# Attention's rows ahead of its keys, the zeroth feature in four runs, a normalisation on ScalarE and two mirrored sums on GpSimd, in a fused attention and two-MLP kernel

## The chip, the cores and the metric

One NeuronCore of a Trainium2 chip runs the kernel. The metric is device microseconds of one execution, median over runs. An engine is named as in the profile: PE is TensorE, PEld its weight loads, DVE is VectorE, ACT is ScalarE, POOL is GpSimd, SP is SyncE, which here only issues transfers.

## The reference, cut to what matters

```python
# attention with decay, B=2, H=8, S=768, D=64, blocks of 64 positions
for b in range(nb):
    intra = einsum(einsum(qb, kb) * Dmask, vb)
    inter = einsum(qb * lam_pow, kv_state)
    out[:, :, sl] = intra + inter
    kv_state = lam_block * kv_state + einsum(kb * rev_pow, vb)
x = out as (B, S, 512)
u = x + real(fft(fft(x, axis=1), axis=2))
x = u + relu(norm(u) @ w_ch1) @ w_ch2            # 512 -> 2048 -> 512
out = x + relu(norm(x) * g_ln @ w_ch1') @ w_ch2'
```

All is float32 from outside. `norm` subtracts the mean of a row and divides by its deviation.

## The kernel before

The program is written out by hand: each engine has one list of instructions in a fixed order, and semaphores join them. An engine that waits holds everything behind it in its list.

**Attention.** Six blocks `c` of 128 tokens, two batches `b`, so 12 units `u = 2c + b`. For a unit PE computes the scores (`scores_of`), DVE multiplies them by the decay mask (`masks`), PE makes the rows (`rows`: the state's part and the masked scores times values; it needs the values, the queries that POOL has multiplied by powers, and the masks), and PE makes keys times values for the state (`keys_values`; it needs POOL's decayed keys `kd`). DVE adds these to the state (`grow_state`), ACT spreads the state (`expand`) and copies the rows out (`x_rows`). In the order before, `keys_values` stands ahead of `rows` in each unit of the loop. SP loads block `c` in two parts, queries and keys (`load_qk`, L301) and keys and values by token (`load_kv`, L304), each 1 MB, and behind each part 512 KB of the first MLP's weights, then the Fourier constants `C1` (L341). PE also runs 11 + 24 matmuls on zeros at the start (L486, L491).

**Fourier stage.** `along(f, c)` (L527) is the transform along the tokens, 16 features of three matmuls each; ACT copies each out (`y_columns`, L848). The column of feature zero is computed apart by small matmuls in `zeroth_feature` (L548), one after each of the 15 `along` of f = 3 to 7, with outputs of 128, 64 or 1 partitions and two columns. `features` (L591) is the transform along the features. DVE forms sums and differences (`differences`) and adds half of them to U (`add_mirrored`, L1202), POOL the other half (`add_rows`, L1581).

**MLPs.** 48 pairs `n`, eight to a stage `s`, six stages: three groups of 512 tokens for each MLP. A pair is seven products of 256 columns (L647), six matmuls each, and 24 matmuls of 512 columns of the second layer (L667) for the pair before it, `down(n - 1, half, t)`. `down(n - 1, 1, 0)` comes right behind the third product of pair n. It waits for the low halves of the second weights of chunk n - 1 (`down_lo`, L1158, on DVE in stage 0) and of the hidden values (`hidden_lo`, L1306). ACT copies the first, seventh and sixth product out (L927, L932, L944), splits weights (`up_hi` L818 and L820, `down_hi` L839) and the next stage's input (`x_hi`, L899), and makes `hidden_hi` (L915). During stage s the input of stage s + 1 is prepared: `statistics`, `deviation` (L864, on ACT), `row_scale`, `normalise` (L1271), in the second MLP also a product with `g_ln` on POOL (`scale_rows`, L1537), then sums (`x_sum`) and the split.

What the program prints for the functions that the diff touches:

## Time and profile before

| | |
|---|---|
| median of 3 runs | 584.7 us (583.88 to 584.91) |
| profiled execution, its own time | 584.5 us |
| its span, first to last instruction | 582.5 us |
| PE busy | 568.9 us, 98% |
| DVE, ACT, POOL busy | 353.3, 242.7, 162.7 us |

The span leaves 2.0 us of the execution outside it. PE is busy for all but 13.6 us of the span. A busy time says that an engine executes, not how much of the array its matmuls use: the small matmuls of the zeroth feature count as the large ones do.

### The profile page before, as it was taken

What the parts mean: (1) busy time and instruction counts of PE and PEld (TensorE: products, weight loads), DVE (VectorE), ACT (ScalarE), POOL (GpSimd) and SP (SyncE); (2) the same over time, 40 slices, a digit from 0 to 9 for tenths busy, and PEclk for the clock granted to TensorE, in tenths of its full rate; (3) what the DMA queues carried; (4) which work ended last, traced back from release to release, by engine and by line L of the source; (5) the groups of instructions that cost most, each with busy time, mean ns of one, the idle gap of its engine ahead of it and who ended that gap; (6) DMA issues with size and microseconds to landing.
All of it is one profiled execution on the core that took longest, in us unless ns stands there. A gap on an engine that the chain in (4) does not pass through costs nothing.

```text
span 582.5 us, 10727 instructions
## 1 busy us (share of the span) xinstructions
PE 568.9 (98%) x4037; PEld 390.6 (67%) x4037; DVE 353.3 (61%) x627; ACT 242.7 (42%) x475; POOL 162.7 (28%) x143
## 2 busy tenths in 40 slices
PE   8999999999899999999999999899999999999997
PEld 4889978666566666666666666566666666666663
DVE  3437788998875775646878676674265433422223
ACT  1255567546663234323546554363222342323231
POOL 1568931763710011003286312620003400000000
PEclk9999999999999999999999999999999999999999
DMA  7999981000137436531235522132000123100001
GB/s 239 393 378 377 351 264 55 2 20 0 37 56 193 132 111 154 136 91 38 74 90 113 141 74 73 36 55 55 19 2 2 37 55 109 73 2 1 0 1 72
DMA packets 78515, 59.85 MB, mean 103 GB/s; under 512 B 39418, under 2 KB 65666, under 8 KB 77060
## 3 DMA queue, kind: packets, MB, share of 16 engines
q1 hardware_dynamic: 76260, 54.49, 32.3%
q10 hardware_dynamic: 1728, 3.15, 1.4%
q0 software_dynamic: 480, 1.57, 0.9%
q8 instruction: 31, 0.51, 0.4%
q14 instruction: 16, 0.13, 0.1%
HBM read 43.73 MB, written 6.30 MB: 86 GB/s over the span
## 4 chain that ended last, share of the span: by engine, by line
PE 77%; DVE 9%; DMA 5%; issue 5%; POOL 3%; ACT 1%; DVEq 0%; SPq 0%; ACTq 0%; POOLq 0%
PE bank L667 36%; PE bank L647 32%; DMA arena<-attn 4%; PE bank L527 2%; PE bank L478 2%; DVE arena L1306 1%; DVE arena L1151 1%; PE bank L473 1%; DVE arena L1149 1%; POOL arena L1479 1%; DVE arena L1158 1%; PE bank L443 1%; PE bank L456 1%; PE bank L591 1%; DVE arena L1271 1%
## 5 line engine op out<-in xcount | busy, mean ns | idle before, releaser
L667 PE MATMUL bank<-arena 128*128 128x512 f16 x1152 | 287.2, 379 | 3.2 <-DVE arena L1158 3.1
L647 PE MATMUL bank<-arena 128*128 128x256 f16 x2016 | 259.3, 273 | 2.7 <-issue 1.9
L647 PEld LDWEIGHTS bank<-arena 128*128 128x128 f16 x2016 | 196.4, 98 | 78.0 <-issue 3.8
L667 PEld LDWEIGHTS bank<-arena 128*128 128x128 f16 x1152 | 112.2, 98 | 90.4 <-DVE arena L1158 3.9
L1306 DVE SCALAR_TENSOR_TENSOR arena<-arena 128x512 f16<-128x512 f32 x96 | 74.2, 773 | 62.4 <-ACT arena L915 62.2
L915 ACT ACTIVATE arena<-arena 128x512 f16<-128x512 f32 x96 | 60.4, 629 | 98.3 <-DVE arena L1353 92.9
L1347 DVE SCALAR_TENSOR_TENSOR arena<-bank,arena 128x256 f32<-128x256 f32 x48 | 20.3, 422 | 65.1 <-PE bank L647 64.7
L1537 POOL TENSOR_TENSOR arena<-arena 128x512 f32<-128x512 f32 x12 | 18.6, 1570 | 90.0 <-DVE arena L1271 90.0
L960 ACT ACTIVATE arena<-bank 128x256 f32<-128x256 f32 x48 | 18.3, 381 | 52.8 <-PE bank L647 52.7
L1283 DVE TENSOR_TENSOR arena<-arena 128x512 f16<-128x512 f32 x42 | 33.0, 796 | 10.1 <-ACT arena L899 10.1
L1353 DVE SCALAR_TENSOR_TENSOR arena<-bank,arena 128x256 f32<-128x256 f32 x48 | 20.2, 421 | 27.4 <-PE bank L647 27.4
L1517 POOL TENSOR_TENSOR arena<-arena 128x256 f32<-128x256 f32 x16 | 14.1, 883 | 80.8 <-DMA arena<-w 64.0
L932 ACT ACTIVATE arena<-bank 128x256 f32<-128x256 f32 x48 | 18.4, 383 | 41.7 <-PE bank L647 41.7
L944 ACT ACTIVATE arena<-bank 128x256 f32<-128x256 f32 x48 | 18.4, 383 | 38.7 <-PE bank L647 38.6
L927 ACT ACTIVATE arena<-bank 128x256 f32<-128x256 f32 x48 | 18.2, 379 | 30.5 <-PE bank L647 30.5
L899 ACT ACTIVATE arena<-arena 128x512 f16<-128x512 f32 x42 | 25.6, 624 | 12.3 <-POOL arena L1537 12.1
L1329 DVE SCALAR_TENSOR_TENSOR arena<-bank,arena 128x256 f32<-128x256 f32 x48 | 20.1, 419 | 17.2 <-PE bank L647 16.8
L478 PE MATMUL bank<-arena 128*128 128x64 f32 x192 | 26.2, 264 | 0.7 <-DVE arena L1034 0.7
L1149 DVE SCALAR_TENSOR_TENSOR arena<-arena 128x1024 f16<-128x1024 f32 x16 | 24.5, 1534 | 2.3 <-ACT arena L818 2.3
L478 PEld LDWEIGHTS bank<-arena 128*128 128x128 f32 x192 | 24.8, 192 | 1.2 <-issue 1.1
L1034 DVE TENSOR_TENSOR arena<-bank,arena 128x512 f32<-128x512 f32 x24 | 15.3, 682 | 13.5 <-PE bank L443 13.5
L1158 DVE SCALAR_TENSOR_TENSOR arena<-arena 128x1024 f16<-128x1024 f32 x16 | 23.2, 1451 | 0.0
(108 smaller groups left out, 527.1 us busy)
## 6 DMA issues: line engine op xcount, KB each, us to landing
arena<-w SPq DMA_DIRECT2D x48, 256.0 KB, 4.3
arena<-w SPq DMA_DIRECT2D x24, 512.0 KB, 4.5
arena<-attn SPq DMA_DIRECT2D x10, 1024.0 KB, 8.9
out<-arena SPq DMA_DIRECT2D x12, 256.0 KB, 2.3
arena<-attn SPq DMA_DIRECT2D x4, 512.0 KB, 4.2
x_near<-arena ACTq DMA_DIRECT2D x6, 256.0 KB, 7.5
x_far<-arena ACTq DMA_DIRECT2D x6, 256.0 KB, 6.2
arena<-c SPq DMA_DIRECT2D x1, 1153.5 KB, 12.1
```

Of the source, the lines that this page charges most:

```text
L478: last = nc.tensor.matmul(xps[b][:, h * D:(h + 1) * D], PT[b][:, par, pair, :], v, start=first, stop=True, skip_group_check=not first)
L647: last = nc.tensor.matmul(bank_, wst[:, i, wx, w, kt, :], xs[s % 2][:, x, ux, :, kt, :], start=not started and k == 0, stop=k == 5, skip_g ...
L667: last = nc.tensor.matmul(ops[t][:], hT[n % 2][:, half, hx, t * P:(t + 1) * P], wdn[:, i, wx, half * DM:(half + 1) * DM], start=first and ...
L899: nc.scalar.activation(hi, block_, ACT.Copy).then_inc(xh_done, 1)
L915: nc.scalar.activation(hT[n % 2][:, half, 0, :], z[n % 2][:, half, :], ACT.Relu).then_inc(hh_done, 1)
L1149: nc.vector.scalar_tensor_tensor(lo[:, 0:1024], sums, scale, hi[:, 0:1024], ALU.mult, ALU.subtract)
L1158: nc.vector.scalar_tensor_tensor(wdn[:, c, 1, :], raw, wscale[:, 2 * m + 1:2 * m + 2], wdn[:, c, 0, :], ALU.mult, ALU.subtract).then_inc(w ...
L1283: nc.vector.tensor_tensor(lo, block_, hi, ALU.subtract).then_inc(xl_done, 1)
L1306: nc.vector.scalar_tensor_tensor(hT[n % 2][:, half, 1, :], z[n % 2][:, half, :], 0.0, hT[n % 2][:, half, 0, :], ALU.max, ALU.subtract).the ...
L1329: nc.vector.scalar_tensor_tensor(z[n % 2][:, 0, 0:HT], chain[1 - n % 2], H_SCALE, p1, ALU.mult, ALU.add).then_inc(z11_out, 1)
L1347: nc.vector.scalar_tensor_tensor(z[n % 2][:, 1, 0:HT], seventh[:, 0:HT], H_SCALE, u2, ALU.mult, ALU.add).then_inc(z21_out, 1)
L1353: nc.vector.scalar_tensor_tensor(z[n % 2][:, 1, HT:TOK], a, H_SCALE, p7, ALU.mult, ALU.add).then_inc(z22_out, 1)
```

## The change

What it does, in the order of the program: the zero matmuls between the first scores and the rows are 21 in place of 24. The mask's two halves arrive on semaphores of their own, the first rows use the first half as soon as it is multiplied, and ACT in place of DVE copies the mask's column `kcol`. In each unit `rows` stands ahead of `keys_values`. The zeroth feature is four runs of three matmuls with four columns each (both batches and both parities at once), behind the `along` of f = 3, 4, 5 and 7, of 128, 128, 128 and 1 output partitions. The columns of `C1` are reordered for it. ACT splits the first half of chunk 1 ahead of `y_columns(5)`, with a wait for `x_out[0]` alone. In stage 0 the two last mirrored sums (j = 4, 5) are on POOL, `down_lo(0, i)` stands directly behind `hidden_lo(n, 1)`, and the input of stage 1 is normalised by ACT in pair 4 (`normal`), as scale times value plus `shift`, a new DVE instruction in `row_scale`. In the stage s = 3 `x_hi` of `X_SECOND` stands behind `hidden_hi(n, 1)` on ACT.

```diff
-WARM_BEFORE, WARM_BETWEEN = 11, 24
+WARM_BEFORE, WARM_BETWEEN = 11, 21
-ZEROTH = ((0, 1, 129, 0, 128, 0), (1, 64, 192, 0, 128, 2), (0, 129, 193, 0, 64, 4), (1, 0, 64, 64, 128, 4),
-          (0, 0, 1, 0, 1, 6))
+ZEROTH = {3: (1, 129, 0), 4: (257, 385, 4), 5: (129, 257, 8), 7: (0, 1, 12)}
...
@@ sync @@
-                             ).then_inc(mask_in, 16)
+                             ).then_inc(mask_in[par], 16)
@@ tensor: rows @@
-                pe.wait_ge(mask_done, 2 * u + 2)
...
+                if first:
+                    for par in range(2):
+                        pe.wait_ge(mask_done, 2 * u + 1 + par)
+                        for pair in range(PAIRS):
+                            last = values(pair, par)
+                else:
+                    pe.wait_ge(mask_done, 2 * u + 2)
...
@@ tensor: the units @@
             rows(0, 0, 0, True)
+            rows(0, 1, 0, True)
             keys_values(0, 0, 0, True)
-            rows(0, 1, 0, True)
...
                     pe.wait_ge(kv_in[slot], 16 * i + 16)
+                    rows(c, 0, slot, False)
                     keys_values(c, 0, slot, False)
-                    rows(c, 0, slot, False)
 
                     scores_of(0, 1 - slot, next_arrived, 4 * c + 2)
+                    rows(c, 1, slot, False)
                     keys_values(c, 1, slot, False)
-                    rows(c, 1, slot, False)
...
@@ tensor: the zeroth feature @@
-            def zeroth_feature(k, c):
-
-                par, lo, hi, first, end, at = ZEROTH[k]
-                return nc.tensor.matmul(bank[7][first:end, at:2 + at], C1[:, c, par * NE + lo:par * NE + hi],
-                                        zeroth_rows[:, par, :] if c == 0 else sfold[(HALF + c) % 2][:, :, par, 0],
-                                        start=c == 0, stop=c == HALF - 1)
+            def zeroth_feature(f):
+
+                lo, hi, at = ZEROTH[f]
+                for c in range(HALF):
+                    if f == 3 and c == HALF - 1:
+                        pe.wait_ge(sf_done, B * HALF)
+                    column = zeroth_rows if c == 0 else sfold[(HALF + c) % 2][:, :, :, 0].rearrange("p b q -> p q b")
+                    last = nc.tensor.matmul(bank[7][0:hi - lo, at:4 + at], C1[:, c, lo:hi], column,
+                                            start=c == 0, stop=c == HALF - 1)
+                if f == 7:
+                    last.then_inc(zeroth_done, 1)
...
                     for c in range(HALF):
                         last = along(f, c)
-                        if f == 3 and c == HALF - 1:
-                            pe.wait_ge(sf_done, B * HALF)
-                        if f < 8:
-                            zeroth = zeroth_feature(f - 3, c)
                     last.then_inc(f1_done, 1)
-                    if f == 7:
-                        zeroth.then_inc(zeroth_done, 1)
+                    if f in ZEROTH:
+                        zeroth_feature(f)
...
@@ scalar @@
+            for par in range(2):
+                act.wait_ge(mask_in[par], 16)
+                last = nc.scalar.activation(kcol.rearrange("p (a r) -> p a r", r=2)[:, :, par], DT[:, par, :, 0], ACT.Copy)
+            last.then_inc(kcol_done, 1)
...
+            def normal(tiles):
+
+                act.wait_ge(shift_done, 1)
+                for t in tiles:
+                    nc.scalar.activation(un[:, t, :], U[:, NT + t, :], ACT.Identity, bias=shift[:, t:t + 1],
+                                         scale=rs[:, t:t + 1]).then_inc(un_done, 1)
...
                 nc.scalar.activation(p1, a, ACT.Copy, scale=H_SCALE).then_inc(p1_out, 1)
...
+                if n == 4:
+                    normal((0, 1))
                 act.wait_ge(p7_done, n + 1)
                 act.wait_ge(z22_out, n)
                 nc.scalar.activation(p7, seventh[:, 0:HT], ACT.Copy, scale=H_SCALE).then_inc(p7_out, 1)
...
+                if n == 4:
+                    normal((2, 3))
                 if prep is not None:
-                    if i == late + 2:
+                    if i == late + 2 and s > 0:
                         deviation(prep)
...
                 nc.scalar.activation(u2, a, ACT.Copy, scale=H_SCALE).then_inc(u2_out, 1)
-                if prep is not None:
+                if n == 3:
+                    deviation(1)
+                if prep is not None and s != GROUPS:
                     for k in X_SECOND[late].get(i, ()):
                         x_hi(prep, k)
...
                 hidden_hi(n, 1)
+                if s == GROUPS:
+                    for k in X_SECOND[late].get(i, ()):
+                        x_hi(prep, k)
...
             y_columns(4)
+            act.wait_ge(x_out[0], 16)
+            up_hi(0, 1, (0,))
             y_columns(5)
             y_columns(6)
-            for b in range(B):
-                act.wait_ge(x_out[b], 16)
-            up_hi(0, 1, (0,))
             y_columns(7)
...
@@ vector @@
-            dve.wait_ge(mask_in, 32)
-            for par in range(2):
-                last = nc.vector.tensor_copy(kcol.rearrange("p (a r) -> p a r", r=2)[:, :, par], DT[:, par, :, 0])
-            last.then_inc(kcol_done, 1)
...
+                    if u == 0:
+                        dve.wait_ge(mask_in[par], 16)
...
+                if s == 1:
+                    dve.wait_ge(ln_step, step + 7)
+                    nc.vector.scalar_tensor_tensor(shift, mv[:, :, 0], -1.0, rs, ALU.mult, ALU.mult).then_inc(shift_done, 1)
...
-                if n == 4:
-                    add_mirrored(5)
...
+                if s == 0:
+                    down_lo(0, i)
                 if prep is not None:
...
                     if i == late + 2:
                         row_scale(prep)
-                        normalise(prep, (0, 1))
+                        if s > 0:
+                            normalise(prep, (0, 1))
                     for k in X_SECOND[late].get(i, ()):
                         x_lo(prep, k)
-                if s == 0:
-                    down_lo(0, i)
...
-                if n == 3:
-                    add_mirrored(4)
...
-                    if i == late + 2:
+                    if i == late + 2 and s > 0:
                         normalise(prep, (2, 3))
...
@@ gpsimd @@
+            def add_mirrored(j):
+
+                pool.wait_ge(ub_in[1], 16 * 6)
+                for half in range(2):
+                    u = U[:, 2 * j + 1, 256 * half:256 * half + 256].rearrange("p (m e) -> p e m", e=2)
+                    last = nc.gpsimd.tensor_tensor(u, u, mirror(DE[DE_SLOT[j]][:, 1 - half, :], half), ALU.add)
+                last.then_inc(addC, 1)
...
             add_rows(4)
+            add_mirrored(4)
             up_sums(0, 5)
             add_rows(5)
+            add_mirrored(5)
             up_sums(0, 6)
```

DVE in pair 3, before, from `hidden_lo(3, 1)` (L1306) on; L1255 to L1264 are `row_scale`, L1271 is `normalise`, L1158 `down_lo`, L1202 `add_mirrored`:

```order
L1306 SCALAR_TENSOR_TENSOR arena<-arena 128x512
L1255 RECIPROCAL arena<-arena 128x4
L1257 TENSOR_TENSOR arena<-arena 128x4
L1259 TENSOR_TENSOR arena<-arena 128x4
L1261 TENSOR_SCALAR arena<-arena 128x4
L1264 TENSOR_TENSOR arena<-arena 128x4
L1271 TENSOR_SCALAR arena<-arena 128x512 x2
L1158 SCALAR_TENSOR_TENSOR arena<-arena 128x1024
L1306 SCALAR_TENSOR_TENSOR arena<-arena 128x512
L1202 TENSOR_TENSOR arena<-arena 128x2x128 x2
L1271 TENSOR_SCALAR arena<-arena 128x512 x2
```

and in the changed kernel, from the same instruction (L1344; L1191 is `down_lo`, L1302 the new `shift`, L1367 the first eviction of pair 4):

```order
L1344 SCALAR_TENSOR_TENSOR arena<-arena 128x512
L1191 SCALAR_TENSOR_TENSOR arena<-arena 128x1024
L1290 RECIPROCAL arena<-arena 128x4
L1292 TENSOR_TENSOR arena<-arena 128x4
L1294 TENSOR_TENSOR arena<-arena 128x4
L1296 TENSOR_SCALAR arena<-arena 128x4
L1299 TENSOR_TENSOR arena<-arena 128x4
L1302 SCALAR_TENSOR_TENSOR arena<-arena 128x4
L1344 SCALAR_TENSOR_TENSOR arena<-arena 128x512
L1367 SCALAR_TENSOR_TENSOR arena<-bank,arena 128x256
```

`down_lo` has moved ahead of `row_scale`; four `normalise` and two halves of a mirrored sum are gone, one small instruction is new.

ACT in pair 4 before, from the copy of the first product (L927); L899 is `x_hi`, L818 and L820 `up_hi`:

```order
L927 ACTIVATE arena<-bank 128x256
L932 ACTIVATE arena<-bank 128x256
L944 ACTIVATE arena<-bank 128x256
L899 ACTIVATE arena<-arena 128x512
L818 ACTIVATE arena<-arena 128x1024
L820 ACTIVATE arena<-arena 128x768
L915 ACTIVATE arena<-arena 128x512
```

and in the changed kernel (L954, L961 and L975 are the copies of the first, seventh and sixth product, L925 is `normal`, L919 `x_hi`):

```order
L954 ACTIVATE arena<-bank 128x256
L925 ACTIVATE arena<-arena 128x512 x2
L961 ACTIVATE arena<-bank 128x256
L925 ACTIVATE arena<-arena 128x512 x2
L975 ACTIVATE arena<-bank 128x256
L919 ACTIVATE arena<-arena 128x512
L834 ACTIVATE arena<-arena 128x1024
L836 ACTIVATE arena<-arena 128x768
```

Two normalisations stand ahead of the copy of the seventh product and two ahead of that of the sixth.

ACT in pair 27 (the fourth pair of stage 3) before, from the copy of the sixth product:

```order
L944 ACTIVATE arena<-bank 128x256
L899 ACTIVATE arena<-arena 128x512
L818 ACTIVATE arena<-arena 128x1024
L820 ACTIVATE arena<-arena 128x768
L915 ACTIVATE arena<-arena 128x512
L960 ACTIVATE arena<-bank 128x256
L915 ACTIVATE arena<-arena 128x512
```

and in the changed kernel:

```order
L975 ACTIVATE arena<-bank 128x256
L834 ACTIVATE arena<-arena 128x1024
L836 ACTIVATE arena<-arena 128x768
L942 ACTIVATE arena<-arena 128x512
L919 ACTIVATE arena<-arena 128x512
L996 ACTIVATE arena<-bank 128x256
L942 ACTIVATE arena<-arena 128x512
```

`x_hi` (L899 before, L919 now) stood ahead of `up_hi` and `hidden_hi` and now stands behind both.

## Rows read from the trace of the kernel before

**Rows 1.** The view of the cores: span and mean granted TensorE clock.

```profile
core 0: 582.5 us, clock 0.999
```

**Rows 2.** Page, part 1: busy us, share and instructions of each engine.

```profile
PE 568.9 (98%) x4037; PEld 390.6 (67%) x4037; DVE 353.3 (61%) x627; ACT 242.7 (42%) x475; POOL 162.7 (28%) x143
```

**Rows 3.** Waits of PE: us in total, times, longest us.

```profile
PE bank L667 <- DVE arena L1158: 3.1, 3, 1.8
PE bank L456 <- POOL arena L1479: 2.0, 5, 0.5
```

**Rows 4.** Timeline of PE, attention: start us, us, what, [idle before].

```profile
1.32 4.21 PE L486 MATMUL bank<-arena 128*128 128x512 f16 x11 [1.32 <-POOL arena L1454]
...
7.45 5.35 PE L491 MATMUL bank<-arena 128*128 128x512 f16 x24
...
15.90 0.69 PE L456 MATMUL bank<-arena 128*64 128x64 f32 x16 [0.48 <-POOL arena L1479]
...
34.77 1.16 PE L443 MATMUL bank<-arena 64*128 64x128 f32 x16
...
53.62 1.16 PE L443 MATMUL bank<-arena 64*128 64x128 f32 x16
...
65.06 3.20 PE L527 MATMUL bank<-arena 128*128 128x193 f32 x18
```

**Rows 5.** Timeline of SP's queue: start us, us of issuing, what.

```profile
22.49 2.38 SPq L301 DMA_DIRECT2D arena<-attn  x1
...
45.48 0.38 SPq L301 DMA_DIRECT2D arena<-attn  x1
...
50.88 2.34 SPq L341 DMA_DIRECT2D arena<-c  x1
```

**Rows 6.** Transfers issued in 22 to 23 us: KB, median us to landing.

```profile
arena<-attn SPq DMA_DIRECT2D x1, 1024.0 KB, 11.4
```

**Rows 7.** The same for 45.2 to 45.6 us.

```profile
arena<-attn SPq DMA_DIRECT2D x1, 1024.0 KB, 7.3
```

**Rows 8.** Page, part 6, the same for the whole span.

```profile
arena<-c SPq DMA_DIRECT2D x1, 1153.5 KB, 12.1
```

**Rows 9.** A window: us, busy PE, PEld, DVE, ACT, POOL; PEclk; DMA share; GB/s.

```profile
30.00:50.00 20.00, 19.17 (x240) 17.82 (x238) 10.04 (x19) 10.99 (x22) 12.46 (x9) 1.00 1.07 373
```

**Rows 10.** Timeline of PE, zeroth feature and after.

```profile
68.50 0.59 PE L527 MATMUL bank<-arena 128*128 128x192 f32 x2
...
71.81 0.57 PE L527 MATMUL bank<-arena 128*128 128x192 f32 x2
...
76.17 0.59 PE L527 MATMUL bank<-arena 128*128 128x192 f32 x2
...
78.56 3.71 PE L591 MATMUL bank<-arena 128*128 128x257 f32 x16 [0.39 <-ACT arena L848]
...
83.15 8.08 PE L527 MATMUL bank<-arena 128*128 128x193 f32 x48
```

**Rows 11.** Timeline of DVE, pairs 2 to 4.

```profile
127.43 1.27 DVE L1240 BATCH_NORM_STATS2 arena<-arena 128x6 f32<-128x512 f32 x2
...
136.52 0.69 DVE L1306 SCALAR_TENSOR_TENSOR arena<-arena 128x512 f16<-128x512 f32 x1
...
138.13 1.00 DVE L1271 TENSOR_SCALAR arena<-arena 128x512 f32<-128x512 f32 x2
139.04 1.28 DVE L1158 SCALAR_TENSOR_TENSOR arena<-arena 128x1024 f16<-128x1024 f32 x1
...
150.31 1.74 DVE L1158 SCALAR_TENSOR_TENSOR arena<-arena 128x1024 f16<-128x1024 f32 x1
```

**Rows 12.** Timeline of PE, the down matmuls of pair 4.

```profile
140.38 0.82 PE L667 MATMUL bank<-arena 128*128 128x512 f16 x3 [0.50 <-DVE arena L1158]
```

**Rows 13.** Timeline of ACT, pair 27.

```profile
375.70 0.63 ACT L899 ACTIVATE arena<-arena 128x512 f16<-128x512 f32 x1 [5.53 <-POOL arena L1537]
```

**Rows 14.** Timeline of PE, pair 28.

```profile
379.08 1.47 PE L647 MATMUL bank<-arena 128*128 128x256 f16 x12 [1.94 <-issue]
```

51 lines of the change are left out of this document (31 added, 20 removed).

## The prediction

> **What bounds the kernel now.** First the view of the cores: the span is 582.5 us at a mean granted clock of 0.999, so TensorE runs at the upper of its two levels, 2.4 GHz [rows 1]. Then the page's first part: PE is busy for 568.9 us of it, 98%, and no other engine for more than 61% [rows 2]. So only two things can shorten the kernel: fewer or cheaper matmuls, or some of the 13.6 us in which PE is idle. The waits of PE name the largest idle pieces: 3.1 us in three waits of the down matmuls for `down_lo`, and 2.0 us in five waits of `keys_values` for POOL's decayed keys [rows 3]. The timelines add three: 1.94 us in pair 28 [rows 14], 0.39 us ahead of `features` [rows 10], 1.32 us at the start [rows 4]; most of the rest lies behind the last matmul, which the change does not touch. The reader should then ask of each piece not who releases it, but what is late next when that releaser is no longer waited for.
>
> **Attention: rows ahead of keys.** The sum of what could go is the 2.0 us of [rows 3], that is 0.48 us in the first unit [rows 4] and about 0.4 in each of four blocks. The wait is for kd, a POOL product of the block's keys, made after the keys land. With `rows` first PE needs only the landing, and POOL works under `rows`. But this stage has a second limit close behind. In 30 to 50 us the DMA engines show a busy share of 1.07 at 373 GB/s [rows 9], and the queue holds a backlog: a queries and keys part issued at 22.49 us [rows 5] lands after 11.4 us [rows 6], at 33.9; PE first uses it at 34.77 [rows 4], 0.9 us later. For the last block it is 45.48 [rows 5] and 7.3 us [rows 7], so 52.8, used at 53.62 [rows 4]: 0.8 us. I take a backlog as the sign that a landing depends on the bytes ahead of it and not on when it is issued; then these landings stay where they are while PE moves up, and the next `scores_of` waits for them. So the gain of the whole stage is capped by that slack, **0.8 us**. The start gains nothing beside it: the split mask and three fewer zero matmuls (24 take 5.35 us [rows 4], 0.22 each, so 0.7) only bring PE earlier to the keys that are at 15.90 now, and these wait for a landing and POOL, which do not move. `C1` lands at 50.88 + 12.1 = 63.0 us [rows 5, 8]; PE would want it at 65.06 - 0.8 = 64.3 [rows 4], so it is not late. Bounds: 0 if PE keeps the transfers' pace with its slack unspent, 2.6 (the 2.0 and 0.6 of the start) if the landings follow PE.
>
> Keys that come behind rows make the state later by the 0.6 to 0.7 us of `keys_values` [rows 4] plus a DVE sum and ACT's copy, but it is used two units later, which is about 9 us (34.77 to 53.62 are four units, 4.7 each [rows 4]). I cost it at nothing. `kcol` on ACT is hidden by the same late keys.
>
> **The zeroth feature.** In [rows 10] the six steps of f = 3 and 4 take 71.81 - 68.50 = 3.31 us, 0.552 each; the next six 76.17 - 71.81 = 4.36, 0.727 each; the last three up to 78.56 - 0.39 = 78.17 take 2.00, 0.667 each. An `along` by itself costs 8.08 / 24 = 0.337 [rows 10]. So a small matmul costs 0.215 with a full output, 0.39 with 64 partitions and 0.33 with one: 1.29 + 2.34 + 0.99 = 4.6 us. Afterwards nine have a full output, 9 x 0.215 = 1.94. Four columns in place of two should cost nothing, since two cost 0.215 and 192 only 0.337. The three with one partition stand at the end and run while PE would wait 0.39 us for ACT anyway; I take 0.5 for the larger of both. So 68.50 to 78.56, 10.06 us, becomes 15 x 0.337 + 1.94 + 0.5 = 7.5: **gain 2.6 us**, 2.0 if the last three cost their 0.33 each and the full ones stop hiding anything, 2.7 at best. ACT's fourth small copy and the earlier half of chunk 1 lie beside this. Everything behind, DVE's chain from `differences(0)` to the first normalisation too, starts from `features` and moves with it.
>
> **Stage 0.** The three waits are 3.1 us: 0.8, 0.50 [rows 12] and 1.8 [rows 3]. In each `down_lo` came last. Now it goes ahead of two statistics (1.27 us [rows 11]) in pair 2. In pair 3 `hidden_lo` is through at 137.1 and `down_lo` began at 139.04 [rows 11]: it can move up by 1.9 us, the wait was 0.50. In pair 4 it ran behind an `x_lo` and, beside POOL, took 1.74 us in place of 1.28 [rows 11]; the DVE work ahead of it is lighter by four normalisations (0.5 each) and two mirrored sums. So most of the three go. What is late next: POOL now has 3 us more of work in pairs 2 and 3, and ACT has four normalisations at the price of an `x_hi`, 0.63 [rows 13] and about 0.55 when they follow each other. They can start only when `shift` is there: 137.1 + 1.2 for `down_lo` + 1.0 for `row_scale` + 0.2 = 139.5. Two take until 140.6, the copy of the seventh product until 141.0. PE would be at the first down matmul at 140.38 - 0.50 - 0.8 = 139.1, and needs that copy three groups of matmuls later, each 3 x 0.22 = 0.66: at 141.0. That is no slack at all, and the second two normalisations before the sixth product's copy are as tight. I put 0.4 us there, 0.4 for what POOL's neighbourhood leaves of the three waits: **gain 2.3 us**, from 3.1 down to 1.3.
>
> At this place a row and a rule meet. The same `down_lo` took 1.28 and 1.74 us [rows 11], the longer one beside POOL. The Trainium skill, "GPSIMD Engine Reference", Specifications, says why: GpSimd shares its SBUF interface with VectorE, and DVE instructions with two SBUF inputs contend. The trace agrees in 0.46 us. By that rule moving two sums to POOL does not free all the DVE time it seems to: it is the third rival.
>
> **Stage 3.** ACT's `x_hi` for the next stage waited 5.53 us for POOL's product with `g_ln`, until 375.70 [rows 13], and held `hidden_hi(27, 1)` and the last copy of pair 27 behind it; PE stood for 1.94 us at the second product of pair 28 [rows 14]. Now `hidden_hi` is ahead. The copy is still behind `x_hi`: it can start at 375.70 + 0.55 = 376.3 and be through at 376.7, and PE needs it where its wait begins, 379.08 - 1.94 = 377.1. **Gain 1.9 us**; bounds 0.5, if something else holds the copy, and 1.94.
>
> **Sum.** 0.8 + 2.6 + 2.3 + 1.9 = 7.6 us. Against the profiled execution's 584.5 that is 576.9; its time is 0.2 us under the median of 584.7, so the forecast is **577.1 us**, by itself within 576.1 to 578.3.
>
> **Rivals.**
> The transfers follow PE (14%): if a landing is a fixed time behind its issue, the 2.6 us are all gained. The two landings that I use took 11.4 and 7.3 us [rows 6, 7], which speaks against a fixed time, as does the busy share of 1.07. 575.3 us.
> Attention gains nothing (12%): the small transfers to DRAM from ACT come earlier and push the loads back by the slack. 577.9.
> Stage 0 gives back (16%): POOL beside DVE delays `down_lo`, `row_scale` and so the normalisations on ACT by 1 us, and PE waits that much at the fourth product of pair 4, and for `down_lo` as before in part. 3.1 shrinks to a gain of 0.9: 578.5.
> The clock falls (6%): in the changed order both units' rows of block 0 are through about 1.5 us before the keys at 15.90, so PE idles there longer than the 0.48 us now [rows 4]. At the start eleven matmuls took 4.21 us, 0.38 each, against 0.22 later [rows 4], so the lower level is near half the pace. If that phase came back for as long, 4.2 us of time would do 2.1 us of work: 577.1 + 2.1 = 579.2. The Trainium skill, "TensorE: Matmul & The Clock Gate", Part 1, warns of exactly this, that an idle PE goes back to half its clock; no row here has an idle piece of that length within the work, so the trace neither agrees nor disagrees.
> The zeroth runs are not cheap (4%): in a run each matmul must load its weights with nothing beside it. If each of twelve costs 0.35, the 2.6 shrinks to 1.0: 578.7.
> The other side (3%): the state is late. If `keys_values` behind `rows` made `grow_state`, `expand` and the next rows of the same batch a chain, every one of the 8 units in blocks 2 to 5 would wait; from 7.6 / 8 = 0.95 us each it eats the whole gain, and at 1.2 us the time is 586.7. The two units between speak against it.
> The forecast has 45%.
>
> **Range and chances.** 574.9 to 580.0 takes in the transfers that follow, stage 0 at its worst and the clock; some 15% stay outside. A measurement of this kernel tells about 0.2% (1.2 us) from no change. Faster by more than that 95%, within it 2%, slower 3%.
>
> **What would show it.** In the trace of the changed kernel: POOL no longer named for `keys_values`, and in its place waits of about 0.4 us of `scores_of` for the transfer of queries and keys in each block; the first `along` at 64.3 us (62.5 if the transfers follow); `features` at 75.1 to 75.3 us; in pair 4 a PE wait under 0.5 us on ACT's normalisations; no wait in pair 28; all other pairs as long as before. A first `along` later than 65.1, a granted clock under 0.99 before 30 us, or a wait over 1 us in pairs 2 to 5 would make it wrong.

## The result, and the profile after

The changed kernel takes **581.54 us** (median of 20 runs, 579.83 to 585.2) against 584.56 us of the kernel before (20 runs beside it); the ratio is 0.9954, with a 95% interval of 0.9943 to 0.9966. That is 2.7 us faster by the ratio, where 7.6 us had been forecast. The profiled execution took 582.56 us, with a span of 580.8 us at a mean granted clock of 0.995, against 582.5 us at 0.999 before [rows 1].

First the page of the changed kernel: the span, the busy times, the granted clock over 40 slices, and one row of the DMA queues.

```profile
span 580.8 us, 10716 instructions
...
PE 567.3 (98%) x4028; PEld 390.7 (67%) x4028; DVE 360.9 (62%) x618; ACT 246.2 (42%) x483; POOL 167.2 (29%) x147
...
PEclk9999999998999999999999999999999999999999
...
q8 instruction: 32, 0.52, 0.4%
```

PE is busy for 1.6 us less than before [rows 2] and idle for 13.5 us, nearly as long as before: waits went, and others came. The tenth digit of PEclk is an 8, where the clock was lower for a time. The mean of 0.995 holds a second such time: from 578.4 us to the end of the span the granted clock is 0.5 as well, but PE's last matmul has ended by then and nothing is slowed. In the kernel before that time is 0.9 us long, here 2.4, since the last output lands later (below).

Now PE's timeline in the places of which the prediction speaks: attention, the zeroth feature and what is behind it, and pairs 3 to 5.

```profile
17.04 1.16 PE L445 MATMUL bank<-arena 64*128 64x128 f32 x16 [0.64 <-DMA arena<-attn]
...
20.83 0.48 PE L486 MATMUL bank<-arena 128*128 128x128 f32 x2 [0.92 <-ACT arena L793]
...
75.40 3.71 PE L602 MATMUL bank<-arena 128*128 128x257 f32 x16 [0.29 <-ACT arena L864]
...
90.11 1.06 PE L643 MATMUL bank<-arena 128*128 128x128 f32 x8 [0.30 <-DVE arena L1309]
...
94.67 0.81 PE L658 MATMUL bank<-arena 128*128 128x256 f16 x6 [0.42 <-DVE arena L1321]
...
134.55 2.14 PE L658 MATMUL bank<-arena 128*128 128x256 f16 x18 [0.28 <-DVE arena L1184]
...
140.94 0.96 PE L658 MATMUL bank<-arena 128*128 128x256 f16 x6 [1.99 <-ACT arena L961]
...
148.47 2.13 PE L658 MATMUL bank<-arena 128*128 128x256 f16 x18
```

`features` starts at 75.40, 3.16 us earlier than at 78.56 [rows 10], and pair 0 at 94.67, 2.66 us earlier than at 97.33. Up to here it is nearly as forecast. But pair 4 then takes 148.47 - 134.55 = 13.92 us, and before it took 10.44 (137.75 to 148.19). In it stands a wait of 1.99 us for ScalarE's copy of the seventh product (L961).

ScalarE and VectorE in pairs 3 and 4 say what the copy stood behind. L925 is `normal`, L1182 and L1184 are `up_lo`, L1191 is `down_lo`, L1290 to L1302 are `row_scale` with `shift` at its end.

```profile
139.09 1.52 ACT L925 ACTIVATE arena<-arena 128x512 f32<-128x512 f32 x2 [3.29 <-DVE arena L1302]
140.52 0.36 ACT L961 ACTIVATE arena<-bank 128x256 f32<-128x256 f32 x1
...
131.24 1.84 DVE L1182 SCALAR_TENSOR_TENSOR arena<-arena 128x1024 f16<-128x1024 f32 x1 [0.33 <-ACT arena L834]
133.01 1.49 DVE L1184 SCALAR_TENSOR_TENSOR arena<-arena 128x768 f16<-128x768 f32 x1
134.42 0.68 DVE L1344 SCALAR_TENSOR_TENSOR arena<-arena 128x512 f16<-128x512 f32 x1
135.02 1.75 DVE L1191 SCALAR_TENSOR_TENSOR arena<-arena 128x1024 f16<-128x1024 f32 x1
136.69 0.17 DVE L1290 RECIPROCAL arena<-arena 128x4 f32<-128x4 f32 x1
136.89 0.48 DVE L1292 TENSOR_TENSOR arena<-arena 128x4 f32<-128x4 f32 x1
137.41 0.65 DVE L1294 TENSOR_TENSOR arena<-arena 128x4 f32<-128x4 f32 x1
138.09 0.17 DVE L1296 TENSOR_SCALAR arena<-arena 128x4 f32<-128x4 f32 x1
138.29 0.57 DVE L1299 TENSOR_TENSOR arena<-arena 128x4 f32<-128x4 f32 x1
138.89 0.17 DVE L1302 SCALAR_TENSOR_TENSOR arena<-arena 128x4 f32<-128x4 f32 x1
```

ScalarE is idle for 3.29 us until `shift` is there at 139.06, then normalises two tiles, and only then copies. GpSimd works beside all of this: its mirrored sums (L1625), and from 134.63 to 138.85 us the four sums of the next chunk of weights, chunk 6 (L1553 to L1558):

```profile
131.26 2.42 POOL L1625 TENSOR_TENSOR arena<-arena 128x256 f32<-128x256 f32 x2
134.63 1.05 POOL L1553 TENSOR_TENSOR arena<-arena 128x256 f32<-128x256 f32 x1 [0.95 <-DVE arena L1184]
135.65 1.71 POOL L1554 TENSOR_TENSOR arena<-arena 128x256 f32<-128x256 f32 x1
137.31 0.72 POOL L1556 TENSOR_TENSOR arena<-arena 128x256 f32<-128x256 f32 x1
138.12 0.73 POOL L1558 TENSOR_TENSOR arena<-arena 128x256 f32<-128x256 f32 x1
```

The three VectorE operations of 0.48, 0.65 and 0.57 us end at 137.37, 138.06 and 138.86, each within 0.03 us of the end of one of these sums (137.36, 138.03, 138.85).

In the kernel before that first sum (L1517) came much later, held by VectorE's mirrored sum of pair 4 (L1202):

```profile
143.68 0.72 POOL L1517 TENSOR_TENSOR arena<-arena 128x256 f32<-128x256 f32 x1 [9.73 <-DVE arena L1202]
```

The busy times by windows show what came behind the wait (behind the window and its length stand PE, PEld, DVE, ACT and POOL, then the granted clock, the DMA share and GB/s).

```profile
138.00:141.50 3.50, 1.51 (x12) 0.82 (x11) 1.89 (x6) 2.41 (x5) 0.77 (x2) 1.00 0.00 0
141.50:144.90 3.40, 3.40 (x14) 1.70 (x12) 0.83 (x3) 3.40 (x6) 1.27 (x1) 0.50 0.00 0
144.90:148.00 3.10, 3.10 (x18) 1.67 (x17) 3.10 (x5) 2.22 (x5) 0.82 (x1) 1.00 0.00 0
```

From 141.49 to 144.91 us the granted clock is 0.5, that is 1.2 GHz: 3.4 us of time for 1.7 us of work.

The last loss is behind the work. PE's last matmul was 3.85 us earlier than before, the end of the span only 1.74 us. These are two rows of the DMA view of the changed kernel around its last output transfer: the queue of instructions with its packets, MB and share, and one transfer's median time from issue to landing.

```profile
q8 instruction: 1, 0.02, 2.1%
...
out<-arena SPq DMA_DIRECT2D x1, 256.0 KB, 4.2
```

And the same view of the kernel before, around its last transfer, where no row of a queue of instructions stands:

```profile
out<-arena SPq DMA_DIRECT2D x1, 256.0 KB, 2.1
```

In the changed kernel a read of 16 KB in the queue of instructions starts at 576.57 us, 0.44 us behind the issue of the last transfer, and takes 1.66 us. The last of the transfer's sixteen parts lands at 580.34, the fifteen others from 578.03 to 578.21. Before, the sixteen landed within 0.18 us.

The profiled execution as a sum (each row but the last is a difference of PE's starts in the two traces):

| part | forecast | measured |
|---|---|---|
| attention, first `along` 65.06 to 64.29 | 0.8 | 0.77 |
| zeroth feature, up to `features` | 2.6 | 2.39 |
| `features` to pair 0 | 0 | -0.50 |
| stage 0, pairs 0 to 5: 62.59 to 63.57 us | 2.3 | -0.98 |
| stage 3, pair 28: 11.92 to 9.76 us | 1.9 | 2.16 |
| behind the last matmul | 0 | -2.10 |
| sum | 7.6 | 1.7 |

### The profile page after: what moved, and what is told of

Read it like the earlier page. It is cut to its first block, busy times and chain, and to the rows that moved or that the text cites. A ratio compares the mean times of both kernels' runs of the same rounds, so it can differ in the third digit from the quotient of the medians.

```text
span 580.8 us, 10716 instructions
## 1 busy us (share of the span) xinstructions
PE 567.3 (98%) x4028; PEld 390.7 (67%) x4028; DVE 360.9 (62%) x618; ACT 246.2 (42%) x483; POOL 167.2 (29%) x147
## 4 chain that ended last, share of the span: by engine, by line
PE 74%; DVE 10%; DMA 5%; issue 4%; POOL 2%; SPq 2%; ACT 1%; DVEq 0%; ACTq 0%; POOLq 0%
PE bank L678 36%; PE bank L658 32%; DMA arena<-attn 5%; PE bank L537 1%; DVE arena L1182 1%; DVE arena L1344 1%; DVE arena L1184 1%; PE bank L475 1%; PE bank L486 1%; PE bank L445 1%; DVE arena L1191 1%; DVE arena L1235 1%; DVE arena L1309 1%; SPq L271 1%; DVE arena L1275 1%
## 5 line engine op out<-in xcount | busy, mean ns | idle before, releaser
L1344 DVE SCALAR_TENSOR_TENSOR arena<-arena 128x512 f16<-128x512 f32 x96 | 73.6, 767 | 59.0 <-ACT arena L942 58.9
L1321 DVE TENSOR_TENSOR arena<-arena 128x512 f16<-128x512 f32 x42 | 33.9, 817 | 10.7 <-ACT arena L919 10.6
L1553 POOL TENSOR_TENSOR arena<-arena 128x256 f32<-128x256 f32 x16 | 15.5, 971 | 74.6 <-DMA arena<-w 64.7
L961 ACT ACTIVATE arena<-bank 128x256 f32<-128x256 f32 x48 | 18.4, 383 | 40.7 <-PE bank L658 40.7
L975 ACT ACTIVATE arena<-bank 128x256 f32<-128x256 f32 x48 | 18.4, 384 | 36.2 <-PE bank L658 36.2
L954 ACT ACTIVATE arena<-bank 128x256 f32<-128x256 f32 x48 | 18.3, 380 | 30.4 <-PE bank L658 30.4
L1367 DVE SCALAR_TENSOR_TENSOR arena<-bank,arena 128x256 f32<-128x256 f32 x48 | 20.1, 419 | 16.5 <-PE bank L658 16.5
L919 ACT ACTIVATE arena<-arena 128x512 f16<-128x512 f32 x42 | 25.6, 622 | 7.2 <-POOL arena L1573 7.2
L1182 DVE SCALAR_TENSOR_TENSOR arena<-arena 128x1024 f16<-128x1024 f32 x16 | 26.9, 1682 | 0.6 <-ACT arena L834 0.6
L1191 DVE SCALAR_TENSOR_TENSOR arena<-arena 128x1024 f16<-128x1024 f32 x16 | 23.7, 1482 | 0.3 <-ACT arena L855 0.3
L1111 DVE TENSOR_REDUCE arena<-arena 128x1 f32<-128x1024 f32 x18 | 21.8, 1211 | 0.7 <-DMA arena<-w 0.7
```

Source lines behind the costliest of these rows:

```text
L919: nc.scalar.activation(hi, block_, ACT.Copy).then_inc(xh_done, 1)
L1111: nc.vector.tensor_reduce(wmax_chunks[:, m, c:c + 1], raw, AX.X, ALU.max, apply_absolute_value=True).then_inc(wred[m], 1)
L1182: nc.vector.scalar_tensor_tensor(lo[:, 0:1024], sums, scale, hi[:, 0:1024], ALU.mult, ALU.subtract)
L1191: nc.vector.scalar_tensor_tensor(wdn[:, c, 1, :], raw, wscale[:, 2 * m + 1:2 * m + 2], wdn[:, c, 0, :], ALU.mult, ALU.subtract).then_inc(w ...
L1321: nc.vector.tensor_tensor(lo, block_, hi, ALU.subtract).then_inc(xl_done, 1)
L1344: nc.vector.scalar_tensor_tensor(hT[n % 2][:, half, 1, :], z[n % 2][:, half, :], 0.0, hT[n % 2][:, half, 0, :], ALU.max, ALU.subtract).the ...
```

## The experiments

All ratios are to the kernel before, run beside each kernel. "Pairs 3, 4, 5" are their lengths in the profiled execution: 10.75, 10.44 and 11.73 us in the kernel before, 10.21, 13.92 and 9.76 in the changed one.

### Four kernels from the changed one

**Normalisations one place later.**

```diff
-                if n == 4:
-                    normal((0, 1))
                 act.wait_ge(p7_done, n + 1)
...
                 if n == 4:
-                    normal((2, 3))
+                    normal((0, 1))
...
                 if n == 3:
                     deviation(1)
+                if n == 4:
+                    normal((2, 3))
```

> The changed kernel with ScalarE's four normalisations of the second stage one place later in pair 4: tiles 0 and 1 behind the copy of the seventh product instead of ahead of it, tiles 2 and 3 behind the copy of the sixth. Theory (W): what the changed kernel loses in pair 4 (13.92 us long against 10.44) is TensorE's wait of 1.99 us for the seventh copy, queued behind normalisations that wait for shift until 139.06, and the granted clock of 0.5 that follows this idle time for 3.41 us and costs about 1.7 us. Then here no wait over 0.7 us stands in pair 4, the clock stays at 1.00 past 141 us, pair 4 takes 10.0 to 10.7 us, and the median is 2.5 to 3.7 us under the changed kernel's, 577.9 to 579.0. Rival (P): GpSimd's work beside VectorE holds up pair 4 whoever normalises; then pair 4 stays over 12 us, and the time within 1 us of the changed kernel's. Rival (C): the clock falls in this stage whatever TensorE waits; then only the 1.99 us come back and a stretch at 0.5 stands somewhere between 125 and 160 us.

Ratio 0.9935 (0.9921 to 0.9950), 580.93 us. Pairs 3, 4, 5: 10.21, 11.74, 10.08. The wait of 1.99 us is gone, the longest in pair 4 is 0.68 us, and the clock is 1.00 in all the work. Of the 3.5 us lost in pair 4, 2.2 came back, and 0.3 were lost again in pair 5. Theory W holds for the wait of 1.99 us, but pair 4 was to be 10.7 at most and the median 579.0 at most: `shift` is as late as in the changed kernel (139.24), and the place on ScalarE does not decide that.

**Stage 0's edits undone, the sums left on GpSimd.** The square root (`deviation`) goes back to its place too.

```diff
-                if n == 4:
-                    normal((0, 1))       # scalar, and normal((2, 3)) behind the copy
...
+                        normalise(prep, (0, 1))      # vector; tiles 2 and 3 later, as before
...
+                if s == 0:
+                    down_lo(0, i)        # behind it, as before
```

> The changed kernel with the edits of stage 0 undone: VectorE normalises the second stage's four tiles in pair 4 ahead of down_lo, as before the change, and ScalarE takes the square root where it did; the mirrored sums of tiles 4 and 5 stay on GpSimd. Theory (W): VectorE's three late down_lo come back (up to 3.1 us of waits in pairs 2 to 5), but not the wait of 1.99 us nor the stretch at a granted clock of 0.5, so that the time is within 1 us of the changed kernel's on either side, 580.5 to 582.5. Rival (P): GpSimd's mirrored sums beside VectorE are the loss; then pair 4 is as long as in the changed kernel or longer, and the time 1.5 to 3 us above it.

Ratio 0.9990 (0.9971 to 1.0008), 2.1 us above the changed kernel's. Pairs 3, 4, 5: 10.74, 14.44, 10.13. These are rival P's numbers: with the sums on GpSimd and a fall of the clock pair 4 is no shorter when VectorE normalises. Its wait is now 2.82 us for `down_lo`, and the clock falls behind it too.

**The mirrored sums back on VectorE.**

```diff
+                if n == 4:
+                    add_mirrored(5)      # vector, pair 4; tile 4 in pair 3
...
-            add_mirrored(4)              # gpsimd
-            add_mirrored(5)
```

> The changed kernel with the mirrored sums of tiles 4 and 5 back on VectorE (pairs 3 and 4), all else as changed. Theory (W): GpSimd's two sums only slow VectorE's up_lo of pair 3 (1.84 and 1.49 us against 1.27 and 1.00) and cost TensorE the 0.28 us at the end of pair 3; with them back VectorE has 1.3 us more work in each of pairs 3 and 4, shift is no earlier, the wait for the seventh copy and the fall of the clock stay, and the time is 0 to 1.5 us above the changed kernel's. Rival (P): the sums on GpSimd are what makes shift late; then shift is done before 138.0, the wait for the seventh copy is under 1 us and the time at least 2 us under the changed kernel's.

Ratio 0.9902 (0.9888 to 0.9917), 579.44 us, 3.0 us better than the changed kernel's ratio (1.7 us better than the ratio of its repetition further down). Rival P held, and what I had theory W expect did not. Pairs 3, 4, 5: 9.77, 11.16, 10.08. The same VectorE instructions, with GpSimd idle:

```profile
135.36 1.28 DVE L1191 SCALAR_TENSOR_TENSOR arena<-arena 128x1024 f16<-128x1024 f32 x1
136.55 0.17 DVE L1288 RECIPROCAL arena<-arena 128x4 f32<-128x4 f32 x1
136.76 0.16 DVE L1290 TENSOR_TENSOR arena<-arena 128x4 f32<-128x4 f32 x1
136.96 0.16 DVE L1292 TENSOR_TENSOR arena<-arena 128x4 f32<-128x4 f32 x1
```

`down_lo` takes 1.28 us and not 1.75, the sums of 4 columns 0.16 and not 0.48 and 0.65. From the start of `down_lo` to the end of `shift` it takes 2.36 us, against 4.04. GpSimd is idle here: its next chunk waits for VectorE's mirrored sum of pair 4 again.

**Nine more instructions on PE.**

```diff
-            for _ in range(WARM_BETWEEN):          # 512 columns each
+            for _ in range(WARM_BETWEEN - 3):
...
+            for _ in range(12):                     # 128 columns each
```

> The changed kernel with nine more instructions for TensorE and no more work: 3 of the 21 zero matmuls of 512 columns at the start are replaced by 12 of 128. In the changed kernel's trace a read of 16 KB in the queue of instructions starts at 576.57 us, behind TensorE's last matmul, and the last output transfer lands 4.2 us after its issue, in the trace before 2.1 us, where no such read stands after 555.6 us. Theory (F): the read comes at a fixed place in TensorE's program, shares one DMA engine with the output and costs the 2.1 us by which the tail has grown; 9 instructions more put the reads elsewhere in time, none stands in the last 6 us, the last transfer lands 2.1 us after its issue, and the median is 1.5 to 2.2 us under the changed kernel's. Rival: the read comes at the program's end wherever the instructions lie, or the slow landing is an accident of one execution; then the tail stays as it is and the median within 0.5 us of the changed kernel's.

Ratio 0.9912 (0.9899 to 0.9925), 579.86 us. No read of instructions stands behind 552.6 us, and the last transfer lands 2.1 us after its issue. In this trace the wait of 1.99 us stands in pair 4 as in the changed kernel, and the clock does not fall behind it; it had fallen at 18.2 us, for 6.8 us, in the middle of a wait of 2.41 us for block 1's queries and keys. So the gain has two parts that this run doesn't separate.

### Repairs together, and waits made on purpose

**Both repairs**: the first and the third edit together.

> The changed kernel with both repairs of stage 0: the mirrored sums of tiles 4 and 5 back on VectorE, and ScalarE's normalisations one place later in pair 4. The first run with the sums back had shift done at 137.8 less its late start, pair 3 9.77 and pair 4 11.16 us long, with waits of 0.53 and 0.20 us in pair 4 behind ScalarE. Theory (M): the sums on GpSimd were what made shift late, and the place on ScalarE matters little once it is early: pair 4 takes 10.4 to 10.8 us here, and the median is 0.3 to 0.8 us under that of the kernel with the sums back alone, a ratio of 0.989 to 0.990 to the kernel before. Rival (W), the place alone matters: the ratio would be that of the kernel with the normalisations late, 0.9935. Rival: the later normalisations make the halves of x in pairs 4 and 5 late; then pair 5 is over 11 us long and the ratio at or over 0.991.

Ratio 0.9913 (0.9897 to 0.9929), 579.3 us. Pairs 3, 4, 5: 9.77, 11.16, 10.08, exactly as with the sums alone; the waits behind ScalarE are gone, and one of another name is there, with this VectorE instruction ahead of it:

```profile
145.44 2.14 PE L658 MATMUL bank<-arena 128*128 128x256 f16 x18 [1.24 <-DVE arena L1184]
...
143.37 2.02 DVE L1184 SCALAR_TENSOR_TENSOR arena<-arena 128x768 f16<-128x768 f32 x1
...
142.32 2.25 POOL L1588 TENSOR_TENSOR arena<-arena 128x512 f32<-128x512 f32 x1
```

Theory M is right that the place on ScalarE matters little once `shift` is early, but pair 4 did not come down to its 10.4 to 10.8 us: `up_hi` on ScalarE stands behind the later normalisations, `up_lo` behind it, and it meets GpSimd's sum that the fourth normalisation releases.

**Both repairs and nine more instructions**: with the fourth edit as well.

> The kernel with both repairs and nine more instructions for TensorE at the start (3 of the 21 zero matmuls of 512 columns become 12 of 128). Theory (F), the read of instructions beside the last output transfer: no read in the instruction queue in the last 6 us, the last transfer lands 2.1 us after its issue, and the time is 1.2 to 2.2 us under that of the same kernel without the nine, run beside it. Rival (no effect, the gain seen with nine more was another chip's or a matter of the granted clock): within 0.5 us of it.

Ratio 0.9906 (0.9888 to 0.9923), 579.43 us: no difference to the kernel without the nine, against theory F. There the read had come at 569.05, ahead of the output. Here three of six runs had a mean clock under 0.999.

**The longer start as well** (the edit is against the kernel just above):

```diff
-            for _ in range(WARM_BETWEEN - 3):
+            for _ in range(WARM_BETWEEN + 1):
...
-            for _ in range(12):
+            for _ in range(8):
```

> The kernel with both repairs, nine more instructions for TensorE as well, but 24 zero matmuls' worth of columns at the start as before the change, instead of 21 (22 of 512 columns and 8 of 128). In two of the traces TensorE waits 1.19 and 2.41 us for the queries and keys of block 1 at about 17 us, and the granted clock is 0.5 from 18.2 us on for 3.4 and 6.8 us; in the trace before it works there without a wait. Theory (S): that wait ends with the transfer, so the 0.65 us of three more zero matmuls hide in it, the wait is 0.65 us shorter and the clock falls in fewer executions: a median 0 to 0.8 us under the kernel with nine more and 21. Rival: block 0's values and not the transfer set what follows, and the 0.65 us come on top: 0.4 to 0.7 us above it.

Ratio 0.9889 (0.9874 to 0.9904), 578.41 us, 1.0 us under the one with 21, and one run of six with a mean clock under 0.999. As theory S has it, a little over its 0.8 us; the intervals overlap.

**Graded waits**, in two runs (the second with pieces of two columns, up to 127):

```diff
+                for k in range(PIECES.get(n, 1) - 1):
+                    nc.scalar.activation(p7[:, 4 * k:4 * k + 4], seventh[:, 4 * k:4 * k + 4], ACT.Copy, scale=H_SCALE)
```

> The kernel with both repairs and nine more instructions, with waits of TensorE made on purpose in eight pairs (9, 14, 19, 26, 31, 35, 39, 43): ScalarE's copy of the seventh product is cut into 8, 11, 14, 18, 22, 28, 36 and 50 pieces instead of one, the work otherwise unchanged. In an undisturbed pair the copy has 1.4 us to spare, so that, at an estimated 0.1 to 0.2 us for a piece, waits of 0 to 8 us come of it, longer from pair to pair. Theory (I): the fall of the granted clock in pair 4 of the changed kernel comes of TensorE's idle time alone: from some length on, each wait is followed within 4 us by a stretch at 0.5, and the waits below it are not; about 2 us lies near that length, since one wait of 1.99 us was followed by a fall and another not. Rival (G): the falls have to do with where in the program or in time they stand; then waits as long as 4 us and more go by at 1.00, or the clock falls where no wait stands.

> Waits of TensorE made on purpose once more, in the same eight pairs of the kernel with both repairs and nine more instructions, longer than at first: ScalarE's copy of the seventh product in 50, 58, 58, 72, 72, 96, 96 and 127 pieces. In the first such kernel 36 and 50 pieces made waits of about 0.9 and 1.8 us, 0.063 us a piece, and the clock stayed up through both; so waits of 1.8, 2.3, 2.3, 3.2, 3.2, 4.7, 4.7 and 6.7 us are due here. Theory (I): idle time alone brings the clock down: every wait over 3 us is followed by a stretch at 0.5 of 3.4 us or more, of those near 2 us some. Rival (G): the falls have to do with place or time; then waits over 3 us go by at 1.00.

In the first the longest of these waits were 0.74 and 1.63 us, and the clock was 1.00 throughout. In the second, PE's timeline behind six of the eight:

```profile
190.98 0.83 PE L661 MATMUL bank<-arena 128*128 128x256 f16 x6 [1.63 <-ACT arena L965]
...
242.11 0.83 PE L661 MATMUL bank<-arena 128*128 128x256 f16 x6 [2.13 <-ACT arena L965]
...
295.76 0.83 PE L661 MATMUL bank<-arena 128*128 128x256 f16 x6 [2.13 <-ACT arena L965]
...
367.31 0.83 PE L661 MATMUL bank<-arena 128*128 128x256 f16 x6 [3.02 <-ACT arena L965]
...
419.57 0.83 PE L661 MATMUL bank<-arena 128*128 128x256 f16 x6 [3.02 <-ACT arena L965]
...
465.02 1.46 PE L661 MATMUL bank<-arena 128*128 128x256 f16 x6 [4.54 <-ACT arena L965]
```

and the windows behind the second to the fifth:

```profile
243.20:246.40 3.20, 3.20 (x12) 1.66 (x11) 1.97 (x4) 0.78 (x2) 0.00 (x0) 0.50 0.44 82
295.80:299.00 3.20, 3.20 (x21) 2.01 (x22) 0.85 (x2) 1.34 (x3) 3.12 (x3) 1.00 0.36 108
367.40:370.60 3.20, 3.20 (x22) 2.00 (x22) 0.85 (x2) 2.61 (x4) 0.00 (x0) 1.00 0.00 0
420.70:424.00 3.30, 3.30 (x12) 1.66 (x11) 0.73 (x3) 0.63 (x1) 0.00 (x0) 0.50 0.00 0
```

Of two equal waits of 2.13 us the first was followed by a fall and the second not; of two of 3.02 us the second and not the first. Behind 4.54 (twice) and 6.50 us the clock fell each time, in the last two for 6.8 us. So idle time brings it down, as in theory I, but not every wait over 3 us did; what told the equal waits of 2.13 and of 3.02 us apart these rows do not show.

### The sums alone, and the fastest kernel

**The mirrored sums on GpSimd alone**, in the kernel before.

```diff
-                    add_mirrored(5)      # vector, and tile 4
...
+            add_mirrored(4)              # gpsimd, behind add_rows(4) and add_rows(5)
+            add_mirrored(5)
```

> The kernel before with one part of the change alone: the mirrored sums of tiles 4 and 5 on GpSimd (two sums each, ahead of the sums for the next block of weights) instead of on VectorE in pairs 3 and 4. Theory (M): this part is what failed. VectorE is relieved of 1.3 us in each of two pairs, but its work beside GpSimd's is slowed, row_scale and down_lo with it, and the three waits for down_lo do not shrink as they should: pair 3 stays at 10.7, pair 4 takes 12.5 us or more against 10.44, and the ratio to the kernel before is 1.002 to 1.006. Rival (A), the part costs nothing by itself and only ScalarE's normalisations make it matter: the ratio is 0.996 to 1.000.

Ratio 1.0003 (0.9984 to 1.0022): missed, no loss that can be measured. Its profiled execution shows the mechanism (pairs 3, 4, 5: 10.74, 14.26, 10.13; a wait of 2.65 us for `down_lo` and a fall behind it), but seven of its twelve runs had a clock of 0.999 or over, and these have spans like the kernel before. So theory M is only half right here, and what the sums themselves cost is settled by the last two kernels below.

**Sums clear of `up_lo`**: both repairs, nine more, the longer start, and in pair 4

```diff
-                if n == 4:
-                    normal((2, 3))
...
                 hidden_hi(n, 1)
+                if n == 4:
+                    normal((2, 3))
+                    # then x_hi of pair 4
```

> The kernel with both repairs, nine more instructions and the longer start, and in pair 4 ScalarE's normalisations of tiles 2 and 3 and its first half of x moved once more, behind up_hi and the first half of the hidden layer. In the trace with both repairs the wait had gone on to the start of pair 5: 1.24 us for up_lo, whose second operation took 2.02 us beside a sum of GpSimd's that the fourth normalisation releases (0.93 to 1.01 in other pairs), and which had started 1.2 us late for want of up_hi. Theory: up_hi goes 1.5 us ahead and the sum comes behind up_lo; the wait of 1.24 us shrinks under 0.4, pairs 4 and 5 take 9.8 to 10.4 and 9.8 to 10.2 us, and the median is 0.8 to 1.4 us under the same kernel without the move, a ratio of 0.9865 to 0.9878 to the kernel before. Rival: the halves of x are late in pair 5 and the wait turns up there: pairs 4 and 5 together stay at or over 21.2 us.

Ratio 0.9859 (0.9824 to 0.9893), **577.03 us**. Pairs 3, 4, 5: 9.76, 9.77, 10.99. The wait is gone from the start of pair 5, and two small ones stand in it, 0.31 and 0.28 us; pair 5 had been expected at 9.8 to 10.2 us and lost 1.2 against the 9.77 of an undisturbed pair. This is called the fastest kernel below.

**Block 0 in the order of before.**

```diff
             rows(0, 0, 0, True)
-            rows(0, 1, 0, True)
             keys_values(0, 0, 0, True)
+            rows(0, 1, 0, True)
```

> The kernel of the run beside it (both repairs, nine more instructions, longer start, sums clear of up_lo) with the first rows of block 0 back in the order of before: rows of unit 0, keys and values, rows of unit 1. Theory (T): block 1 starts when its queries and keys have landed, whatever the order, so that this is worth under 0.3 us in an execution in which the granted clock stays up; but TensorE idles in one piece for the transfer at about 17 us only where the order of block 0 leaves it nothing to do, and the stretches at 0.5 near 18 us come of that. Then the mean granted clock is at 0.999 or over in more of the runs here than beside it. Rival: the falls at 18 us come with the landing alone; then as many runs have a mean clock under 0.998.

Ratio 0.9870 (0.9839 to 0.9900). Two runs of six had a mean clock under 0.999, beside it none of five. There is no sign of theory T: its profiled execution idles 1.61 us for POOL in block 0 and the clock falls at 18.4 us all the same.

### The tail and the share of falls

The first is the fastest kernel with `WARM_BETWEEN` matmuls of 512 columns (21) and none of 128; the second is the fastest unchanged.

> The fastest kernel so far (both repairs, sums clear of up_lo) with the start of the changed kernel: 21 zero matmuls of 512 columns and not the nine instructions more. Beside it runs the same kernel with them. Theory (F), the read of instructions beside the last output transfer: a read stands behind 565 us here and none there, the last transfer lands about 4.2 us after its issue in the traces in which the read starts inside the last microsecond before or after that issue, and the median is 1 to 2.2 us above that of the kernel beside it. Rival: no difference over 0.5 us.

> The fastest kernel so far once more (both repairs, nine more instructions, longer start, sums clear of up_lo), on the chip of the three others. Both theories on the tail expect its first result again: ratio 0.985 to 0.988 to the kernel before, mean granted clock at 0.999 or over in most runs, no read of instructions in the last 6 us.

Without the nine instructions (and with the short start) 0.9892 (0.9868 to 0.9917), 578.69 us; with them 0.9881 (0.9857 to 0.9905), 578.10 us. The repetition lies just over the 0.985 to 0.988 that was expected of it. The difference of 0.6 us is no more than the longer start brought by itself above (1.0 us), so theory F's 1 to 2.2 us in the median are not there. In the trace without the nine a read stands at 577.52, behind the last landing.

The changed kernel with the second and the third edit together:

> The changed kernel with all of stage 0 as before the change: VectorE normalises and adds the mirrored sums of tiles 4 and 5, down_lo behind the normalisations. What is left of the change is attention's order, the zeroth feature's four runs and the order of x_hi in stage 3. Sum of theory (M), read from the traces: 2.7 us at the start of pair 0 and 2.1 in pair 28, less 2.1 for the tail where the read of instructions meets the last transfer: 582.5 less 2.7 is a span of 577.8 to 579.9, a ratio of 0.991 to 0.996, so that the changed kernel's stage 0 as a whole brought nothing or cost up to 2 us. Rival: stage 0 as changed is still worth something; then the ratio here is over the changed kernel's.

Ratio 0.9953 (0.9921 to 0.9985), 581.76 us; span of the profiled execution 578.0 at a clock of 1.00; pairs 0 to 5 take 62.66 us. That is inside theory M's ranges. The ratio is above that of the changed kernel beside it (0.9931, next), as the rival has it, with overlapping intervals; in the two profiled executions the changed stage 0 is worth 0.35 us (62.66 against 62.31).

And without any edit:

> The changed kernel itself, on the chip of the three others. Theory (W and C together): the wait of 2.0 us in pair 4 stands in every execution and the fall of the clock behind it in most: the mean granted clock is under 0.999 in more than half of the runs, and the ratio 0.994 to 0.997. Rival: the fall was an accident of the profiled execution; then most runs are at 0.999 or over.

Ratio 0.9931 (0.9893 to 0.9968), 579.75 us. Three of six runs are at 1.000 and three under 0.999, which decides neither for the theory nor for the rival. The profiled execution has the same wait of 1.99 us, **no fall** (mean clock 1.000) and no read before its last landing, and a span of 577.3 us:

```profile
140.87 0.83 PE L658 MATMUL bank<-arena 128*128 128x256 f16 x6 [1.99 <-ACT arena L961]
```

It is the changed kernel undisturbed: 5.2 us under the kernel before.

### The mirrored sums, or what held GpSimd back

> The changed kernel, with one wait more: GpSimd's sums for chunk 6 of the first weights (four operations, 4.2 us) wait for shift. In the kernel before they wait for VectorE's mirrored sum of tile 5 in pair 4 and start at 143.68, when row_scale is long done; in the changed kernel nothing holds them, and they run at 134.56 to 138.77 beside down_lo, row_scale and shift. Theory (N): not the mirrored sums but these four operations, released early by the part moved to GpSimd, make shift late. Then down_lo takes 1.28 us here and the small operations 0.17, shift is done at 137.4 to 137.9 (with pair 0 at 94.6), pair 4 takes 11.0 to 11.4 us, and an undisturbed execution has a span of 575.8 to 576.4 us; ratio 0.989 to 0.991. Rival: the mirrored sums themselves and what they have pushed back do it; then shift is at 138.5 or later and pair 4 over 12 us.

```diff
                         pool.wait_ge(addC, 2)
+                        pool.wait_ge(shift_done, 1)
```

Ratio 0.9905 (0.9871 to 0.9939), 578.91 us. Pairs 3, 4, 5: 10.21, 10.94, 9.77. PE's wait and the VectorE rows behind it (pair 0 starts 0.93 us later here than in the changed kernel, behind a fall of the clock at 18.0 us):

```profile
140.17 0.83 PE L658 MATMUL bank<-arena 128*128 128x256 f16 x6 [0.61 <-ACT arena L961]
...
135.94 1.27 DVE L1191 SCALAR_TENSOR_TENSOR arena<-arena 128x1024 f16<-128x1024 f32 x1
...
137.34 0.16 DVE L1292 TENSOR_TENSOR arena<-arena 128x4 f32<-128x4 f32 x1
137.53 0.16 DVE L1294 TENSOR_TENSOR arena<-arena 128x4 f32<-128x4 f32 x1
```

Theory N held: one wait on GpSimd makes `shift` 1.7 us earlier and takes 1.4 us from PE's wait, with the mirrored sums where the change put them (pair 4 and the spans of the two runs at 1.000, 575.4 and 575.5 us, came out slightly under what was expected). Counted from the start of pair 0, `shift` is still 0.54 us later than with the sums on VectorE: `up_lo` takes 1.84 and 1.50 us beside them here, and 1.28 and 1.01 there. That is the mirrored sums' own share.

> The fastest kernel so far (normalisations behind the copies and clear of up_lo, nine more instructions, longer start), but with the mirrored sums of tiles 4 and 5 on GpSimd as in the change, and GpSimd's sums for chunk 6 held until shift. Theory (N): the part is harmless once its successor is held, and VectorE is 1.5 us lighter in each of two pairs: pairs 3, 4, 5 together take 30.3 to 30.8 us (30.5 in the fastest so far), the ratio is 0.985 to 0.988, no difference that can be measured. Rival: GpSimd's chunk 6 comes too late for the products of pair 6; then a wait over 0.5 us stands in pair 5 or 6 and the ratio is over 0.989.

Ratio 0.9873 (0.9848 to 0.9899), 577.58 us; pairs 3, 4, 5: 10.21, 9.78, 10.22. As expected, no difference to the fastest that can be measured.

## Why the prediction was wrong

**Attention, right.** 0.77 us of 0.8; the waits for queries and keys are there in four places (0.64 us the longest), POOL is no longer named. One thing was not in it: the first rows of block 1 wait 0.92 us for `expand` (L793), the late state, which I had costed at nothing. It came out of the slack to the transfers: block 2's scores still wait 0.31 us for theirs at 33.70.

**Zeroth feature, right to 0.2 us**, `features` at 75.40 for 75.1 to 75.3. That everything behind moves with it was wrong by 0.5: VectorE's chain to the first normalisation ended 2.44 us earlier and not 3.16, since in 70 to 78 us it still had `up_lo` and a maximum to do, and PE waits 0.30 us for it at 90.11, where it did not wait before; the 0.42 us ahead of pair 0 stood there before too.

**Stage 0, the step that failed.** The prediction had 2.3 us, with "0.4 for what POOL's neighbourhood leaves" and "0.4" for ScalarE's normalisations (its "from 3.1 down to 1.3" is a slip: 3.1 - 2.3 leaves 0.8). Undisturbed it was 0.28 us (62.59 to 62.31 in the second profile of the changed kernel), so 2.0 were missing. The place was right: `shift`, two normalisations, the copy, "no slack at all". The term that failed is the time at which `shift` is there. In the time of the kernel before (2.66 us later) it came at 141.7, not 139.5: `hidden_lo` was through at 137.8 and not 137.1 (`up_lo` beside the mirrored sums), `down_lo` took 1.7 for 1.2 and `row_scale` with `shift` 2.4 for 1.2, both beside the sums of chunk 6. Of the lateness, the repairs show 1.7 us to come of the sums of chunk 6 and 0.5 of the mirrored sums. A smaller term was off as well: the two normalisations took 1.43 us up to the start of the copy (139.09 to 140.52) and not 1.1. The sums of chunk 6 had been held by a VectorE instruction that the change takes away: I had listed GpSimd's added work and not what it would start earlier. The rival "Stage 0 gives back" named VectorE beside GpSimd and put 1 us on the normalisations' delay; `shift` was 2.2 us late.

The four combinations, as ratios to the kernel before. In the left column `down_lo` stands behind the normalisations, in the right ahead of `row_scale`, so that the columns differ in that too:

| | VectorE normalises | ScalarE normalises |
|---|---|---|
| mirrored sums on VectorE | 0.9953 (0.9921 to 0.9985) | 0.9902 (0.9888 to 0.9917) |
| mirrored sums on GpSimd | 0.9990 (0.9971 to 1.0008) | 0.9954 (0.9943 to 0.9966), again 0.9931 (0.9893 to 0.9968) |

The right column is better by 3.0 us in the upper row and by 2.1 or 3.4 in the lower, as the step wanted; which part of it is the normalisations' and which `down_lo`'s place no run shows. The sums on GpSimd cost 2.2 us in the left column and 3.0 or 1.7 in the right, falls of the clock included, by runs that were not all made side by side; in the kernel before by themselves they cost nothing that can be measured (1.0003). With the sums on VectorE pairs 0 to 5 take 60.68 us, 1.91 less than before, and 60.57 with them on GpSimd and the next chunk held: the stage's 2.3 us were nearly there.

The rule of the Trainium skill that I weighed there, "GPSIMD Engine Reference", Specifications, is that GpSimd and VectorE share their SBUF interfaces, and that VectorE instructions with two SBUF inputs or in a 2-port mode contend. The trace agrees in the changed kernel's small operations with two inputs, which take 0.48, 0.65 and 0.57 us, and in the reciprocal with its one input, 0.17 beside a GpSimd sum. The operation with a constant took 0.17 here, where it started 0.03 us ahead of a sum, and 0.66 with stage 0's edits undone, where it started behind one; which mode it ran in no row tells. I had priced the rule from one row, 0.46 us on an instruction of 1.28. In these rows a small operation lasts until the sum beside it ends, and the next one meets the next sum, so a chain of small ones loses far more of its time: 0.16 became 0.65.

**The clock.** The rival had it fall in block 0, at 6%. It fell in pair 4 in this profiled execution, behind the 1.99 us, and cost 1.26 us there (63.57 against 62.31). In 19 of 26 runs of the changed kernel the mean clock was under 0.999, in 10 of 68 of the kernel before. That is no exact count of falls in the work: in the profiled execution the time at 0.5 behind the last matmul alone takes 0.002 off the mean. At 0.997 or under, where the profiled executions with a stretch of 3.4 us in the work lie, were 13 of the 26 and 9 of the 68. So falls are part of why the median is over the undisturbed execution. They are not all of it: the four of the 20 runs at 0.999 have spans of 578.0 to 580.6 us. It also fell at 18 to 24 us in five of the eighteen experiments' traces, so the place that the rival named is real. The Trainium skill, "TensorE: Matmul & The Clock Gate", Part 1, says that an idle PE goes back to half its clock. The traces agree, and a wait of 2 us was followed by it. The prediction said that no row had an idle piece of the length in question, which was some 2 us; [rows 14] has one of 1.94 us, and the clock did not fall behind it.

**Stage 3, right**: 2.16 us for 1.9.

**The tail** was in no step. Its 2.10 us are those of the profiled execution: a read of instructions ran beside the last output transfer. That read stands in all nine traces with the changed kernel's count of PE instructions, at 569 to 579 us, and in three of them it ran beside the last transfer; only in these did the sixteen parts of it land far apart (2.31, 2.12 and 1.85 us, else under 0.2). With nine more it stands near the end of none of nine traces; the count does not decide it alone, since with the sums alone in the kernel before, which has the same count as those nine, a read stands at 585.68, behind the last landing. In the medians of the one pair run side by side for it this was worth at most 0.6 us.

The sum for the undisturbed execution: 7.6 - 2.02 (stage 0) - 0.63 (start of the pairs at 94.56, 2.77 and not 3.4 earlier) + 0.26 (stage 3) = 5.2, the measured 582.5 - 577.3. What the 20 runs lack beyond that, 2.2 us by the medians and 2.5 by the ratio, was in no term of the sum. Falls of the clock and late landings are in it, both seen in the profiled execution; how much each has, and what else there is, stays open, as only span and mean clock are known of the other runs.

## What to carry to other kernels

When work goes from VectorE to GpSimd, price it by the VectorE chain that GpSimd will then run beside, with all that GpSimd starts earlier for it. Before a helper gets work ahead of a copy on which TensorE depends, add up when its operand is ready in the changed kernel, slowed as it will be, and put the work behind the copy; and ask what an engine that is relieved had been holding back. A wait of 2 us on TensorE cost 3.3 where the clock fell behind it, and 2 where it did not: look at the granted clock of all runs, not of the profiled one alone, and take off what falls behind the last matmul.

## What the runs showed of the hardware

- The same wait of 1.99 us at the same place was followed by 3.4 us at 1.2 GHz in one execution of the changed kernel and by none in another, nor in the kernel with nine more instructions. Waits of 2.82 and 2.65 us for `down_lo` were followed by a fall. Of waits made on purpose, those up to 1.63 us never brought a fall, 2.13 and 3.02 us each once in two, 4.54 (twice) and 6.50 each time. At the start of attention, where several waits stand close together, it fell beside single waits of 0.99 and 1.19 us and within one of 2.41, and did not beside one of 2.45 (the last kernel).
- The queue of instructions reads 16 KB at a time, in the MLPs once in 14 to 24 us. In the three traces in which a read stood beside the last output transfer of 256 KB, one sixteenth of that transfer landed 1.7 to 2.1 us behind the others, and the span was that much longer.
- Operations of 4 columns with two inputs on VectorE took 0.16 to 0.17 us alone and 0.48 to 0.65 beside GpSimd, each until the end of the sum beside it; one of 768 columns 1.00 and 2.02. Sometimes GpSimd was the one slowed: from 124.38 us in the changed kernel a sum (L1553) took 2.25 us, where the one at 134.63 took 1.05, and the `down_lo` beside it at 124.77 took its usual 1.27.
